# Three reorderings around the last chunk of a fused attention, MLP and routed-expert kernel

## What is computed

```python
x = attention(q, k, v)            # window of 64, (4*576, 512)
h = x @ w_in                      # 512 -> 2048
g = h * tanh(log1p(exp(h)))
x = g @ w_out                     # 2048 -> 512
go = x @ w_skip > 0               # these tokens are computed, the others pass
logits = x @ w_gate               # 8 experts
e = argmax(logits);  gate = softmax(logits)[e]
out = x;  out[go] = x + gate * (relu(x @ w1[e]) @ w2[e])   # 512 -> 1024 -> 512
```

## Time and profile before

| | us |
|---|---|
| median of 3 runs | 697.94 (696.72 to 699.56) |
| the profiled execution's own time | 698.9 |
| its span, first to last instruction | 697.3 |
| PE busy | 674.3 |
| DVE busy | 492.5 |
| ACT busy | 358.2 |
| POOL busy | 254.6 |

### The profile page before, as it was taken

One profiled execution on the slowest core, in us unless ns is written; L12 is line 12 of the kernel. 1 busy time (PEld: TensorE's weight loads), 2 busy tenths in 40 slices (PEclk: granted clock), 3 DMA queues, 4 the chain that ended last, 5 costly groups with the idle time before them and its releaser, 6 DMA issues. The chain is left out here.

```text
span 697.3 us, 14240 instructions
## 1 busy us (share of the span) xinstructions
PE 674.3 (97%) x5234; PEld 591.3 (85%) x5234; DVE 492.5 (71%) x968; ACT 358.2 (51%) x784; POOL 254.6 (37%) x230
## 2 busy tenths in 40 slices
PE   7799999999999999999999999999999999999994
PEld 6776888888888888889888988887888988899894
DVE  5897778876877786886786687689589745464361
ACT  5556566565555555555456556544554243533530
POOL 3322343444352453353343344344543331221221
PEclk9999999999999999999999999999999999999998
DMA  9834131162164242134115114002647899999940
GB/s 273 254 91 151 50 96 39 39 104 70 42 112 90 72 75 63 43 60 112 39 47 129 39 39 108 31 8 56 242 157 265 236 399 390 357 330 357 352 156 2
DMA packets 62884, 97.20 MB, mean 139 GB/s; under 512 B 23062, under 2 KB 27158, under 8 KB 62816
## 3 DMA queue, kind: packets, MB, share of 16 engines
q1 hardware_dynamic: 59200, 91.01, 43.1%
q0 software_dynamic: 3168, 4.51, 2.1%
q10 hardware_dynamic: 448, 0.79, 0.4%
HBM read 84.97 MB, written 13.73 MB: 142 GB/s over the span
## 5 line engine op out<-in xcount | busy, mean ns | idle before, releaser
L1642 POOL TENSOR_TENSOR q_sb<-n_sb,r_sb 128x512 f32<-128x512 f32 x72 | 94.1, 1307 | 277.1 <-ACT r_sb L945 160.9
L677 PE MATMUL Y<-wout_hi,g_hi 128*128 128x512 f32 x272 | 111.2, 409 | 3.0 <-ACT g_hi L951 2.8
L649 PE MATMUL H<-x_hi,win_hi 128*128 128x256 f32 x384 | 111.9, 291 | 1.3 <-DVE x_lo L1153 1.3
L649 PE MATMUL H<-x_hi,win_lo 128*128 128x256 f32 x384 | 108.5, 283 | 0.0
L649 PE MATMUL H<-x_lo,win_hi 128*128 128x256 f32 x384 | 108.5, 282 | 0.0
L677 PE MATMUL Y<-wout_lo,g_hi 128*128 128x512 f32 x272 | 107.5, 395 | 0.0
L1648 POOL TENSOR_TENSOR g_lo<-g_sb,g_hi 128x512 fp32r<-128x512 f32 x68 | 88.2, 1297 | 2.2 <-ACT g_hi L951 1.7
L781 PEld LDWEIGHTS H<-xT,w 128*128 128x128 f32 x768 | 87.6, 192 | 1.0
L781 PE MATMUL H<-xT,w 128*128 128x128 f32 x768 | 88.0, 275 | 0.0
L649 PEld LDWEIGHTS H<-x_hi,win_hi 128*128 128x128 f32 x384 | 73.0, 190 | 6.0 <-issue 3.6
L677 PE MATMUL Y<-wout_hi,g_lo 128*128 128x512 f32 x272 | 75.6, 399 | 0.0
(11 more groups left out here) (212 smaller groups left out, 1418.5 us busy)
## 6 DMA issues: line engine op xcount, KB each, us to landing
w<-moe_w SPq DMA_DIRECT2D x23, 2048.0 KB, 10.4
kT<-k_T SPq DMA_DIRECT2D x32, 256.0 KB, 3.1
vw<-v_w SPq DMA_DIRECT2D x32, 256.0 KB, 3.2
y_rows<-ytile SPq DMA_DIRECT2D x36, 128.2 KB, 7.2
out_rows<-ytile SPq DMA_DIRECT2D x36, 128.0 KB, 2.9
win<-moe_w_in SPq DMA_DIRECT2D x8, 512.0 KB, 8.8
qbd<-q_T SPq DMA_DIRECT2D x64, 64.0 KB, 2.6
wout<-moe_w_out SPq DMA_DIRECT2D x8, 512.0 KB, 7.3
```

The source lines that it names most:

```text
L649: last = nc.tensor.matmul(HM3[J % 3][:, f, :], wt[:, j, d, f * P:(f + 1) * P], xt[:, c % 2, d, :], start=(n == 0), stop=(n == 3 * DB - 1))
L677: last = nc.tensor.matmul(Y[t][:, :], gt[:, J % 2, lo:lo + P], wt[:, 2 * j + f, :], start=(j == 0 and f == 0 and wt is wout_hi and gt is g ...
L1642: nc.gpsimd.tensor_tensor(q_sb[:, :], n_sb[:, J % 2, :], r_sb[:, J % 2, :], ALU.mult).then_inc(q_ok, 1)
```

## The change

In the steps from J = 62 on (`g_leads`), DVE does a, b, c of J before n(J+1), ACT does g_hi(J) before r(J+1) (and so before `y_out_of_psum` and `y_T_out` of that tick), and POOL does g_lo(J) before q(J+1). In chunk 8 the two copies of the logits on DVE stand one step later. The first two early experts are picked at once in step 61 (`pick_two`), before `gate_and_row` of step 62, so from counts that lack chunk 6; `taken` is still made from the counts with chunk 6, now in step 63 (`held_by_two`).

```diff
-        PSTEPS = 12
+        PSTEPS = 13
...
+        def g_leads(J):
+
+            return J >= (NC - 1) * NJ - 2
...
+                if g_leads(J):
+                    g_hi_out(J)
                 if ahead:
                     mish_recip(J + 1)
                 if c > 0 and j == 0:
                     y_out_of_psum(c - 1)
                 if route_at(c, j) == 2:
                     y_T_out(c - 1, 1)
-                g_hi_out(J)
+                if not g_leads(J):
+                    g_hi_out(J)
...
-            def pick_first():
-
+            def pick_two():
+
+                dve.wait_ge(ex_ok, NC - 2)
                 step, count = steps(picked, 0)
                 held = df[:, 0, :]
                 step(nc.vector.tensor_tensor(held, nextrow[:, :], ecap[:, :], ALU.subtract))
                 nc.vector.tensor_copy(basev[:, 0:NE], ecap[:, :])
                 nc.vector.tensor_scalar(enov[:, 0:NE], rev[:, 0, :], -1.0, float(NE), ALU.mult, ALU.add)
                 nc.vector.memset(dv[:, :], 0.0)
-                nc.vector.tensor_scalar(taken[:, :], held, float(P), None, ALU.min)
                 marked(0, step)
                 strike(0, step)
-                assert count[0] == 6, count
-
-            def pick_second():
-
-                step, count = steps(picked, 6)
                 marked(1, step)
...
                 step(nc.vector.tensor_tensor(early[:, :], ohe[:, 0, :], ohe[:, 1, :], ALU.add))
-                step(nc.vector.tensor_tensor(taken[:, :], taken[:, :], early[:, :], ALU.mult))
-                assert count[0] == PSTEPS - 6, count
+                assert count[0] == PSTEPS - 2, count
+
+            def held_by_two():
+
+                step, count = steps(picked, PSTEPS - 2)
+                held = df[:, 0, :]
+                step(nc.vector.tensor_tensor(held, nextrow[:, :], ecap[:, :], ALU.subtract))
+                step(nc.vector.scalar_tensor_tensor(out=taken[:, :], in0=held, scalar=float(P), in1=early[:, :],
+                                                    op0=ALU.min, op1=ALU.mult))
...
+                if g_leads(J):
+                    mish_g(J)
                 if J < NC * NJ - 1:
                     mish_n(J + 1)
                 if gp:
                     normalise(*gp)
-                mish_g(J)
-                if route_at(c, j) == 0:
-                    logits_out(c - 1, 0)
-                if route_at(c, j) == 2:
-                    logits_out(c - 1, 1)
+                if not g_leads(J):
+                    mish_g(J)
+                late = 1 if c == NC - 1 else 0
+                for t in range(TT):
+                    if route_at(c, j) == 2 * t + late:
+                        logits_out(c - 1, t)
...
+                if c == NC - 2 and j == 5:
+                    pick_two()
                 if c == NC - 2 and j == 7:
-                    pick_first()
-                if c == NC - 1 and j == 0:
-                    pick_second()
+                    held_by_two()
...
+                if g_leads(J):
+                    g_lo_out(J)
                 if J + 1 < NC * NJ:
                     mish_q(J + 1)
-                g_lo_out(J)
+                if not g_leads(J):
+                    g_lo_out(J)
```

More of the change, by code:

```diff
@@ L1331, in pick_second @@
                 step(nc.vector.tensor_tensor(early[:, :], ohe[:, 0, :], ohe[:, 1, :], ALU.add))
-                step(nc.vector.tensor_tensor(taken[:, :], taken[:, :], early[:, :], ALU.mult))
-                assert count[0] == PSTEPS - 6, count
+                assert count[0] == PSTEPS - 2, count
[5 more added lines that the diff above has]
+                                                    op0=ALU.min, op1=ALU.mult))
+                assert count[0] == 2, count
             def pick_third():
```

## The result

| | before | after | difference |
|---|---|---|---|
| first runs, median of 4 each | 698.75 us | 712.23 us (711.15 to 720.54) | ratio 1.0231, 95% interval 1.0168 to 1.0293 |
| more runs on another chip, median | 697.6 us (27) | 714.57 us (6; 712.11 to 716.28) | ratio 1.0233, 1.0204 to 1.0262 |
| span of the first profiled execution | 697.3 us | 719.0 us | |
| its granted clock | 0.994 | 0.980 | |
| blocks | 12 | 13 | |

The kernel is slower by 2.3%. The four first executions have their median at 712.2, 13.5 over before and near the forecast of 711.7; six more have it at 714.6, above the range of 709.3 to 713.8. The difference to the kernel before, 17.0 us in the larger set (714.57 - 697.6), is 3.2 us more than the forecast's 13.8. Three of the first four ran at a mean granted clock of 0.994 to 0.997, the six at 0.988 to 0.995, so that the first median came so near is in part luck.

The account below looks back on a forecast made before the run. PE, busy for 97% of the span, was taken to bound the kernel by its own list of work. Block 13.16 + scatter 0.4 + last chunk 0.2 = +13.8 us on 697.94 gave 711.7 us, range 709.3 to 713.8 (8 in 10).

Parts of the forecast that it names:

- 12 blocks before, 13 after, +13.16 us: Expert blocks in the tail: picks from older counts give one block more, at 13.16 us a block.
- Rivals 1 and 2: Rival 1: still 12 blocks, 698.1 us, chance 0.03; rival 2: 12 blocks, leads win all 4 us, 694 us, 0.02.
- Last scatter +0.4: End of the kernel: the last scatter carries 75 rows instead of 13, adding 0.4 us.
- jump back 0: Loop's second working pass, for the 13th block: the jump back is hidden and costs 0, bound 1.2 us.
- pick_two and steps 62 and 63: Last chunk: pick_two out at 467.4, down_hi(62) at 470.2 (+0.9 us), gate_and_row ends 473.9, down_hi(63) at 476.7.
- down_hi(64) ... starts at 484.8 instead of 482.69: +2.1 us: Step 64: down_hi(64) waits for the copies of Y behind r(65), +2.1 us, bounds 1.5 and 3.0.
- the bound of 3.0: Step 64: upper bound of the +2.1 us, if held_by_two is caught behind q(64) and holds a(64).
- "-1.9 us" behind it: After step 64: PE's waits of steps 66, 68 and 70 go, 0.36 + 0.76 + 0.77 = -1.9 us.
- the leading steps' own pace: From step 65: g, n, r, q, b and c in turn need 5.2 us, under PE's shortest step of about 5.7.
- The clock: PE's granted clock: 0.994 of full speed in the old profile; the sum has no term for a fall.
- Rival 4: 13 blocks, and the chunk loses 3 us or the jump back shows: 714 to 715 us, chance 0.07.

Follow-up runs that it names:

- the choice of experts: Kernel before, order untouched, expert 6 set aside in the first two picks so 13 blocks follow: 711.31 us beside 698.12, ratio 1.0189.
- the late copies alone: Kernel before with only the copies of the logits of chunk 7 a step later: 697.90 us beside 698.77, ratio 0.9982.
- the fillers: Changed order, 12 blocks, plus 44 unused products at step 64, then also 28 before block 3's transposes: 701.53 and 700.15 us, beside 702.80 without.

## Why the prediction was right and where it failed

- *12 blocks before, 13 after, +13.16 us:* right. Measured 13.19 us in the chain and 13.2 us in the median with the choice of experts (with 0.4 us of that edit's own). The counts of the inputs, borne out by the sizes of three scatters, carried the forecast; no row of the last chunk shows it. Rivals 1 and 2 are out.
- *Last scatter +0.4, jump back 0:* the landing took 0.37 us more, as forecast, but the span has nothing of it (9.2 us behind PE's last product either way). The jump back shows nowhere.
- *pick_two and steps 62 and 63:* right to 0.2 us (467.4, 470.3, 474.0, 476.9 by the old time).
- *"down_hi(64) ... starts at 484.8 instead of 482.69: +2.1 us":* this step failed. It was +3.3, over the bound of 3.0, for g(64) ended 1.1 us later than the sum had it. held_by_two, caught behind POOL, was in the bounds and not in the sum, and without it q(64) beside a(64) costs nearly the same.
- *"-1.9 us" behind it:* the waits of 66, 68 and 70 did go, 1.6 us in all where the clock stayed up. The cause I gave was wrong in half: the late copies alone take away the waits of 66 and 68 and give the whole 1.6 us, and the leading steps' own pace is 5.9 and not 5.2 us. Of these 0.7 us 0.5 is q beside a (1.78 and not 1.30 us).
- *The clock:* this step failed too; it was put at nothing. I took PE's products at their old length behind a wait longer than any in the old trace's last chunk. In four of five profiled executions the clock was at half for 3 to 7 us, and steps 64 to 71 took 1.1 to 2.3 us more than the 44.96 of the fifth. Rival 4, the chunk loses 3 us, came nearest.
- The sum that the runs show: 13.2 for the block, nothing for the scatter, 3.3 - 1.6 for waits, and up to 2.3 for the clock, 14.9 to 17.2 us; measured 17.0.
- *Open:* how much exactly of the 3.8 to 4.2 us that the order costs is the clock. Waits explain 1.7 to 1.9; the fillers took back 1.3 and 2.7 us of the median, with overlapping intervals; the estimate from the mean clocks is 1.5 to 1.9. Why the gather of block 3 is late in two of the profiled executions (3.5 and 4.0 us) and not in the others was not tried.

## What to carry to other kernels

When a change makes a decision from older data, work out the decision on the real inputs before any timeline: here one comparison, 112 against 105 tokens, cost 13 us and outweighed every wait that was being tuned. An order in which each result is finished before the next is begun shortens one latency, but puts the parts of one step in a row and beside each other; compare that row's length with the bottleneck's step, and look at what else (here the copies of Y and y_T_out) has moved behind it. And when the bottleneck is a PE at full clock, price a wait of several microseconds at more than its length.

## What was not expected of the hardware

- The granted clock of PE fell to half after a wait of 2.9 to 3.3 us within the busiest part of the kernel (0.50 from 486 to 492 us), in some executions and not in others with the same wait, and in the three profiled executions with products filling it not there. In the kernel with the new picks alone it fell after a wait of 1.86 us.
- POOL's q, 128x512 elements, took 1.78 us where DVE's a on the same two tiles had begun just before it, and 1.3 otherwise; in the kernel with held_by_two behind g(64), q(65) began first, and a(65) took 1.80 us where it takes 0.69.
- Many of DVE's operations of 8 columns took 0.9 to 2.8 us where POOL was busy, ending with one of POOL's instructions, and 0.15 to 0.23 us otherwise. Its reductions were not held: one took its usual 0.16 us at 482.83 in the kernel before, in the middle of POOL's g_lo (482.73 to 484.02).
